# The row of negated maxima in a tiled attention: six narrow matmuls with a repeated column as stationary operand, or diagonals made by Pool and two wide ones

## The reference

```
mask   = q_assign[:, :, :, None] == k_assign[:, :, None, :]     # nearest of 16 centroids, by argmax
scores = scale * np.matmul(q, k.transpose(0, 1, 3, 2))
scores = np.where(mask, scores, -1000000000.0)
scores = scores - np.max(scores, axis=-1, keepdims=True)
attn   = np.exp(scores)
attn   = attn / (np.sum(attn, axis=-1, keepdims=True) + 1e-09)
return np.matmul(attn, v)
```

## Time and profile before

| | |
|---|---|
| median of 3 runs | 881.55 us (879.17 to 884.61) |
| profiled execution, first to last instruction | 883.2 us (the page gives this span as its only time) |
| granted clock of TensorE, mean | 0.952 |
| PE busy | 799.7 us, 91% |
| DVE, ACT, POOL busy | 383.8, 300.6, 175.7 us |
| attention stage | about 7 to 315 us of the span |

### The profile page before, as it was taken

How to read it: one execution, slowest core, us unless ns; L and a number is a source line. 1 busy time by engine, 2 the same in 40 slices (tenths; PEclk the granted TensorE clock), 3 DMA queues, 4 the chain that set the end, 5 groups by cost and what they waited for, 6 DMA issues and landing times. The chain is left out here.

```text
span 883.2 us, 14341 instructions
## 1 busy us (share of the span) xinstructions
PE 799.7 (91%) x5357; PEld 749.7 (85%) x5358; DVE 383.8 (43%) x660; ACT 300.6 (34%) x467; POOL 175.7 (20%) x209
## 2 busy tenths in 40 slices
PE   4889999999999970988999998767999999999998
PEld 4789999999999960877889997657999898989896
DVE  4625444454454154545556663217424251515050
ACT  1434343443443240535445554225222131303020
POOL 2212212212211053000000000007313141404050
PEclk9889999999999995899999998796999999999999
DMA  5647657657647525466655652604000000000000
GB/s 117 135 96 169 138 126 163 144 121 169 139 90 216 159 74 193 156 223 240 240 209 183 219 203 95 238 26 143 1 24 2 24 0 24 0 24 0 24 1 24
DMA packets 77823, 100.96 MB, mean 114 GB/s; under 512 B 44616, under 2 KB 44616, under 8 KB 77768
## 3 DMA queue, kind: packets, MB, share of 16 engines
q1 hardware_dynamic: 74408, 89.20, 36.0%
q0 software_dynamic: 3360, 11.01, 3.5%
HBM read 59.30 MB, written 20.45 MB: 90 GB/s over the span
## 5 line engine op out<-in xcount | busy, mean ns | idle before, releaser
L500 PE MATMUL psVD<-Vp,PT 128*128 128x128 f32 x1152 | 148.4, 276 | 0.0
L500 PEld LDWEIGHTS psVD<-Vp,PT 128*128 128x128 f32 x1152 | 144.6, 192 | 0.5
L782 DVE TENSOR_REDUCE neg_max<-psM 128x1 f32<-128x768 f32 x90 | 86.2, 957 | 73.5 <-PE psM L474 73.5
L1475 PE MATMUL psS<-xe_hi,w_hi 128*128 128x256 f32 x384 | 110.0, 286 | 1.4 <-DVE xe_lo L1421 1.4
L1440 DVE TENSOR_SCALAR tmin<-psS,alpha_c 128x256 f32<-128x256 f32 x96 | 46.4, 484 | 147.1 <-PE psS L1477 146.9
L1476 PE MATMUL psS<-xe_lo,w_hi 128*128 128x256 f32 x384 | 109.9, 286 | 0.0
L1477 PE MATMUL psS<-xe_hi,w_lo 128*128 128x256 f32 x384 | 109.8, 286 | 0.0
L652 ACT ACTIVATE PT<-psS 128x768 f32<-128x768 f32 x96 | 76.4, 811 | 87.5 <-PE psS L492 87.5
L1362 POOL TENSOR_TENSOR g_lo<-gf,g_hi 128x256 fp32r<-128x256 f32 x96 | 70.8, 739 | 177.0 <-ACT g_hi L1399 177.0
L1120 DVE TENSOR_TENSOR w_lo<-raw,w_hi 128x1024 fp32r<-128x1024 f32 x78 | 92.4, 1220 | 31.1 <-ACT w_hi L1115 31.0
L1026 PE MATMUL psS<-xe_hi,w_hi 128*128 128x256 f32 x256 | 75.7, 296 | 12.8 <-issue 11.1
(11 more groups left out here) (188 smaller groups left out, 1325.2 us busy)
## 6 DMA issues: line engine op xcount, KB each, us to landing
raw<-in_moe_w SPq DMA_DIRECT2D x16, 2048.0 KB, 10.5
xs_slots<-zero SPq DMA_DIRECT2D x8, 832.0 KB
K<-Kh SPq DMA_DIRECT2D x32, 192.0 KB, 2.9
xe_n<-xs_slots SPq DMA_DIRECT2D x16, 256.0 KB, 9.8
ys_slots<-y_sb POOLq DMA_DIRECT2D x16, 256.0 KB, 5.7
raw<-in_moe_w_in SPq DMA_DIRECT2D x2, 2048.0 KB, 8.7
raw<-in_moe_w_out SPq DMA_DIRECT2D x2, 2048.0 KB, 11.5
Qn<-in_q SPq DMA_DIRECT2D x16, 192.0 KB, 5.1
```

Of the source, the lines that this page charges most:

```text
L500: mm = pe.matmul(psV[:, PVS * t:PVS * t + P], PT[par][:, c, t * P:(t + 1) * P], Vp[par][:, c, :], start=(c == 0), stop=(c == T - 1))
L782: nc.vector.tensor_reduce(neg_max[:, t:t + 1], ps[t % 2][:, 0:2, 0:HALF], AX.XY, ALU.max, negate=True).then_inc(s_nm, 1)
L1475: pe.matmul(o, w_hi[:, w], xe_hi[:, c, :], start=(c == 0), stop=False)
```

## The change

The columns of neg_max become stationary operands themselves: for each tile one column, repeated 128 times by a stride of zero, is multiplied with an identity in fp32r. Each output row is again the row of negated maxima, 128 values for each matmul. neg_max is therefore of type fp32r, `ident_r` takes the place of `ones_r`, and DVE copies it from the identity at the start. Pool's diagonals, their buffer and their semaphore go.

```diff
-        ones_r = sb("ones_r", [P, P], F32R)
+        ident_r = sb("ident_r", [P, P], F32R)
...
-        diag = sb("diag", [P, T, P], F32R)
-        neg_max = sb("neg_max", [P, T])
+        neg_max = sb("neg_max", [P, T], F32R)
...
             def max_row(g):
-                for h in range(2):
-                    pe.wait_ge(s_dg, 2 * g + h + 1)
-                    mm = pe.matmul(psM[:, h, 0:HALF], ones_r[:, :],
-                                   diag[:, 3 * h:3 * h + 3, :], start=True, stop=True)
+                for t in range(T):
+                    pe.wait_ge(s_nm, T * g + t + 1)
+                    col = (t % 3) * P
+                    mm = pe.matmul(psM[:, t // 3, col:col + P], neg_max[:, t:t + 1].broadcast_to([P, P]),
+                                   ident_r[:, :], start=True, stop=True)
                 mm.then_inc(s_bc, 1)
...
-            pe.wait_ge(s_const, 2)
+            pe.wait_ge(s_const, 1)
+            pe.wait_ge(s_idr, 1)
             pe.wait_ge(s_qk, 64)
...
+            dve.wait_ge(s_const, 1)
+            nc.vector.tensor_copy(ident_r[:, :], ident[:, :]).then_inc(s_idr, 1)
             nc.vector.memset(wg[:, :, :], 0.0).then_inc(s_wg0, 1)
...
             def maxima(g, guard, onehots_of=None, ps=(psM, psM)):
                 for t in range(T):
-                    if guard and t % 3 == 0:
-                        dve.wait_ge(s_dg, 2 * g - 1 + t // 3)
+                    if guard and t == 0:
+                        dve.wait_ge(s_bc, g)
...
-                           allow_small_or_imprecise_dtypes=True)
+                           allow_small_or_imprecise_dtypes=True).then_inc(s_const, 1)
...
-            nc.gpsimd.memset(ones_r[:, :].bitcast(F32), 1.0).then_inc(s_const, 1)
...
-            def diagonal(g, guard):
-                for h in range(2):
-                    half = slice(3 * h, 3 * h + 3)
-                    pool.wait_ge(s_nm, T * g + 3 * h + 3)
-                    if guard and h == 0:
-                        pool.wait_ge(s_bc, g)
-                    nc.gpsimd.tensor_tensor(diag[:, half, :],
-                                            ident[:, :].unsqueeze(1).broadcast_to([P, 3, P]),
-                                            neg_max[:, half].unsqueeze(2).broadcast_to([P, 3, P]),
-                                            ALU.mult).then_inc(s_dg, 1)
-
             lo_parts(0, True)
-            diagonal(0, False)
             lo_parts(1, False)
 
             def body(j, prev, nxt, nxt2):
-                diagonal(2 * j + 1, True)
-                if nxt:
-                    diagonal(2 * j + 2, True)
                 if nxt2:
                     lo_parts(j + 2, False)
```

More of the change, by code:

```diff
@@ L198, in program @@
         s_nm = sem("s_nm")
-        s_dg = sem("s_dg")
+        s_idr = sem("s_idr")
         s_bc = sem("s_bc")
```

## The result

The changed kernel takes 902.94 us (900.52 to 903.5, 4 runs) against 882.82 (879.17 to 884.61, 4 runs): a ratio of 1.0231, 95% interval 1.0189 to 1.0273. It is 20 us slower.

What follows compares the result with a forecast made beforehand. PE was taken to bound the attention stage, busy in all of 100 to 280 us. Heads 2 to 15 at +4.5 us less 0.2 for heads 0 and 1 gave +4.3 on 881.55: 885.9 us, range 880.5 to 895.5.

Steps and rivals of the forecast that it cites:

- I pass a change of the stage on to the end one for one: Attention stage hands over serially to routing, scatter and experts, so its change in time reaches the end in full.
- (a): Present pair of 384-column matmuls in PE's stream: costs 0.35 to 0.43 us a head.
- (b): Six 128-column matmuls in PE's stream: 0.112 us each, set by the load, together 0.75 us, +0.32 a head.
- the full fp32 price: Rival: narrow fp32r matmuls cost as plain fp32, 0.22 us for 128 columns, 895.4 us in all; chance 0.17.
- (c): Heads 2 to 15, all in a full PE: 14 x 0.32 = +4.5 us, bounds +0.1 and +13.9.
- (d): ACT's copy of the row goes 0.28 us later, still covered before PE's next use; costs no time.
- (g): Six PE waits for tile maxima where two were: all met long before, 0 taken, at most 5.6 us.
- (h): Pool loses 32 operations of 0.83 us, which delayed nobody from 64 us on: zero.
- (i): At the start, DVE's fp32r identity copy, some 0.3 us, is hidden because PE's first transposes wait for their DMA.
- (e): Head 0, diagonals on the path: ACT's copy starts 0.48 us earlier, 0.4 us of gain left at full clock.
- (f): Head 1, PE waits for ACT's one-hots: six matmuls add 0.32 us; 0.2 us gain taken for heads 0 and 1 together.
- The rival of the clock: Rival: one half-clock stretch at 33 or 46.7 us is not entered, winning up to 3.4 us, 882.5 us; chance 0.08.

Runs made afterwards that it cites:

- after_plus192: Changed kernel with 192 instructions (met waits) added where PE idles after the second token count: 886.81 us, ratio 1.0038.
- row_of_64_columns: Changed kernel with each head's six matmuls streaming 64 columns instead of 128, half the row not made: 902.39 us in one run.
- before_plus192: Kernel before the change with 192 instructions (met waits) added where PE idles after the second token count: 873.87 us, ratio 0.9899.
- before_plus224: Kernel before the change with 224 instructions added in PE's idle place: 881.33 us, ratio 0.9962.
- skipped_plus64: Kernel before the change with 64 never executed instructions added in expert 0's jumped-over overflow code: 896.52 us, ratio 1.0141.
- before_plus64: Kernel before the change with 64 instructions (met waits) added in PE's idle place: 899.14 us, ratio 1.0158.
- before_plus128: Kernel before the change with 128 instructions added in PE's idle place: 910.65 us, ratio 1.0292.
- skipped_plus192: Kernel before the change with 192 never executed instructions added in expert 0's jumped-over overflow code: 875.14 us, ratio 0.9901.
- after_plus128: Changed kernel with 128 more instructions added in PE's idle place: 879.8 us, ratio 0.9938.
- two_narrow_rows_plus176: Kernel before the change with six narrow matmuls in heads 0 and 1 only, plus 176 instructions: 876.29 us, ratio 0.9901.
- two_narrow_skipped_plus176: Kernel before the change with six narrow matmuls in heads 0 and 1 only, plus 176 never executed instructions in expert 0's overflow code: 872.08 us, ratio 0.9884.

## Why the prediction was wrong

**The step that failed** is the sentence "I pass a change of the stage on to the end one for one". It put the length of the later stages at unchanged, without a term for it. The hand-over itself held (25.9 and 26.0 us from the second token count to the first expert product), the length of what follows didn't. The later stages are executed from a program that the change makes longer, and the experts' stage, which jumps over some 650 instructions at the end of each expert, depends on where its code stands: +16.0 us of the 17.9, and back to -0.3 when 192 more instructions restore the place (after_plus192). I counted the instructions of the change for their time on PE's array and never for their place. The rows to ask existed: the page's line of 36 instruction packets, and 14.2 us of waits on "issue" at the expert products, in a kernel whose experts were otherwise dense. They should have been a rival of their own, with the bounds that the runs now give: 7 us to be gained and 25 to be lost by placement alone. The range had nothing from outside the attention.

**(a), (b), the price of a narrow matmul: right.** 0.112 us was forecast, and the starts stand 0.113 apart. Six with the unhidden first load cost 1.97 - 1.69 = 0.28 more than the pair in the slot shown, against a forecast of 0.32; over the 13 steps from head 2's row to head 15's it is 3.9 / 13 = 0.30. row_of_64_columns shows that the streamed columns don't set it; the load does by the argument of (b). The 81 ns of the Trainium skill (TensorE: Matmul & The Clock Gate, "Back-to-back issue gap"), weighed in (b), didn't hold here, and the full fp32 price didn't either.

**(c): right.** 14 x 0.30 = 4.2 us for 4.5.

**(d), (g), (h), (i): right.** PE has no wait from 55 to 290 us, ACT's copy starts 0.28 us later behind the row's first matmul (0.91 for 0.63), as forecast, and delays nobody, and Pool's busy time fell from 175.7 to 147.1 us for nothing. The six waits cost nothing that stamps show. PE's first transposes still wait for their DMA.

**(e): right in size** (0.46 us for 0.48). **(e) and (f) together: right at equal clock.** From start to the row of head 2 it took 64.3 us before and 61.1 after, but kernels with the same attention as before took 59.4 to 64.3, and such with narrow rows in every head 61.1 to 63.7. In each, two stretches of granted clock 0.5 fall between these rows (a third lies ahead of head 0's), of 3.4 us in some executions and of 6.8 in others. From the row of head 0 to that of head 2 the kernels sort by that:

| both stretches | pair of 384 columns | six of 128 columns |
|---|---|---|
| 3.4 us | 30.87 to 30.89 us (before_plus192, before_plus224, skipped_plus64) | 30.66 (after) |
| 6.8 us | 33.14 to 33.38 (before, before_plus64, before_plus128, skipped_plus192) | 33.19 (after_plus128), 33.20 (two_narrow_rows_plus176) |

(Two more with narrow rows, after_plus192 and two_narrow_skipped_plus176, have one stretch of each length and take 31.45 and 31.58; row_of_64_columns is left out.) So by single executions the narrow rows gain 0.1 to 0.2 us here, where 0.2 was forecast, and the shorter stretches 2.4 us. The rival of the clock was a true one, but it belongs to the execution more than to the change: both lengths stand in both columns. The 3.2 us that the result's pair of profiles shows is luck for the most part.

**Not foreseen, small:** +2.4 us from head 15's row to the second token count. The row itself accounts for about 0.3. In the routing a stretch at the lower clock appears, 320 to 324 us at 0.69:

```profile
320.00:324.00 4.00, 4.00 (x27) 4.00 (x26) 0.36 (x1) 2.87 (x4) 3.08 (x4) 0.69 0.56 214
```

Before it was 1.00 there:

```profile
320.00:324.00 4.00, 4.00 (x38) 4.00 (x38) 2.16 (x3) 3.92 (x6) 3.08 (x4) 1.00 0.51 197
```

It follows on the short idle times of PE at the barrier, which both kernels have. It isn't the only cause of such a loss: after_plus192 and row_of_64_columns have it and take 48.9 us too, but after_plus128 takes 48.5 without it, and three kernels with the pair in these heads (before_plus128, before_plus224, two_narrow_rows_plus176) take 48.2, also without it, where PE waits 1.9 us for DVE's copy of the transposed tokens. What decides between 46.5 and 48 us stayed open.

**The change alone**, at equal placement, costs 2.9 us (886.81 against 883.88, interval 1.9 to 4.7), where the working had 4.3. The forecast of it holds; the 16.0 us that it left out in the experts' stage are more than five times the measured 2.9.

## What to carry to other kernels

Where PE's program jumps or loops while DMAs are busy, an edit anywhere ahead of it moves its code against the blocks in which instructions are fetched, and that alone was worth -1% to +3% here. Before the gain or loss of an edit is believed, compare at equal placement (fill up to a multiple of 256 instructions, or read the waits on "issue" and the packets of the instruction queue beside the time); filling with instructions that never run is also a cheap thing to tune, and 192 of them made this kernel 1% faster. For small products in a full PE, count the matmuls, each with its load of 128 stationary columns, at 0.11 us each up to 128 columns, and not streamed columns.

## What was not expected of the hardware

A wait for instructions can be long: gaps of 10 to 12 us at one jump with the DMA engines busy at about 1.00 and 385 GB/s ahead of it, against 1 us at others. The packets themselves took 1.7 and 1.9 us of the 10.17; why the rest is so long isn't shown. A matmul with 64 streamed columns takes as long as one with 128. And a stationary operand that repeats one column by a stride of zero loads like any other (190 ns as recorded, 191 for the matrix of ones).
